# A mask, a scan and the matmul order of the attention loop, moved on four engines

## The reference, cut to what matters

```python
for t in range(S):                       # S = 768; B*H = 32 heads of D = 48
    cur = einsum('bhd,bhe->bhde', u * k[t], v[t])
    y[t] = einsum('bhd,bhde->bhe', r[t], state + cur)
    state = w[t][..., None] * state + einsum('bhd,bhe->bhde', k[t], v[t])
x = y.transpose(0, 2, 1, 3).reshape(B * S, H * D)     # 3072 x 384
x = moe(x)          # skip gate, argmax over 8 experts, relu(x @ w1) @ w2
return moe2(x)      # softmax over tokens and over slots, 8 experts
```

## Time and profile before

| What | us |
|---|---|
| three runs | 380.25, 381.19, 381.48 |
| median | 381.19 |
| profiled execution: its span, first to last instruction | 387.5 |
| attention, to the first transpose of a token tile (L637) | 138.3 |
| one pair of attention once the loop has settled | 8.10 |

### The profile page before, as it was taken

One profiled execution on the slowest core, in us unless ns is written; L12 is line 12 of the kernel. 1 busy time (PEld: TensorE's weight loads), 2 busy tenths in 40 slices (PEclk: granted clock), 3 DMA queues, 4 the chain that ended last, 5 costly groups with the idle time before them and its releaser, 6 DMA issues.

```text
span 387.5 us, 14814 instructions
## 1 busy us (share of the span) xinstructions
PE 354.1 (91%) x5880; PEld 269.6 (70%) x5880; DVE 281.8 (73%) x564; ACT 221.0 (57%) x681; POOL 115.0 (30%) x179
## 2 busy tenths in 40 slices
PE   6699999999999999889999999999999999679990
PEld 6487777877777788656777777777777777345360
DVE  7999999999999634786676767777677776430371
ACT  3777888778887755134656556565555664200060
POOL 3543322343223340254222233332221224540000
PEclk9989999999999999989999999999999999689996
DMA  8987656766568995013193799495858779759438
GB/s 310 415 305 265 241 198 216 257 258 248 197 205 286 424 402 205 3 23 111 29 393 128 300 323 393 178 361 193 325 211 321 263 259 396 281 170 327 167 152 336
DMA packets 31300, 97.58 MB, mean 252 GB/s; under 512 B 4062, under 2 KB 14410, under 8 KB 29722
## 3 DMA queue, kind: packets, MB, share of 16 engines
q1 hardware_dynamic: 29466, 93.81, 65.2%
q0 software_dynamic: 1792, 3.17, 2.7%
HBM read 85.53 MB, written 11.45 MB: 250 GB/s over the span
## 4 chain that ended last, share of the span: by engine, by line
PE 56%; DVE 5%; another core or an unknown queue 3%; issue 1%; POOL 1%; ACT 1%; DVEq 0%; ACTq 0%
PE a_bank L772 19%; PE y_bank L781 18%; PE y_bank L928 3%; PE a_bank L944 3%; PE a_bank L637 2%; DVE x_all L1550 2%; PE sums_bank L705 1%; PE a_bank L832 1%; PE y_bank L598 1%; PE y_bank L593 1%; PE ktok_bank L645 1%; PE sums_bank L645 1%; PE y_bank L605 1%; PE y_bank L740 0%
## 5 line engine op out<-in xcount | busy, mean ns | idle before, releaser
L781 PE MATMUL y_bank<-w_sb,work 128*32 128x192 f32 x1664 | 78.5, 326 | 0.5 <-ACT work L1131 0.5
L772 PE MATMUL a_bank<-w_sb,work 128*32 128x256 f32 x1248 | 77.9, 382 | 0.1
L781 PEld LDWEIGHTS y_bank<-w_sb,work 128*32 128x32 f32 x1664 | 64.9, 110 | 8.8 <-DVE work L1396 1.1
L1586 POOL TENSOR_SCALAR_AFFINE_SELECT a_sb<-a_sb 128x512 f32<-128x512 f32 x48 | 44.2, 932 | 86.7 <-ACT a_sb L1016 86.7
L772 PEld LDWEIGHTS a_bank<-w_sb,work 128*32 128x32 f32 x1248 | 42.4, 109 | 25.6 <-issue 13.0
L1026 ACT ACTIVATE bonus_v<-v_sb,bonus 128x48 f32<-128x48 f32 x192 | 45.0, 321 | 14.0 <-DVE x_all L1260 13.9
L1104 ACT ACTIVATE work<-work 32x96 f32<-32x96 f32 x108 | 30.4, 281 | 39.3 <-PE a_bank L772 37.0
L1440 DVE TENSOR_TENSOR ys<-work 32x192 f32<-32x192 f32 x104 | 37.0, 355 | 9.9 <-ACT work L1131 9.2
L1396 DVE STREAM_TRANSPOSE work<-hid 128x256 f32<-128x256 f32 x53 | 23.6, 446 | 26.2 <-PE y_bank L781 22.9
L572 PE MATMUL a_bank<-r_in,k_in 64*128 64x128 f32 x384 | 31.0, 295 | 0.1
L572 PEld LDWEIGHTS a_bank<-r_in,k_in 64*128 64x128 f32 x384 | 24.7, 193 | 6.3 <-issue 5.7
(11 more groups left out here) (314 smaller groups left out, 582.6 us busy)
## 6 DMA issues: line engine op xcount, KB each, us to landing
w_sb<-in_moe_w SPq DMA_DIRECT2D x20, 1536.0 KB, 11.7
wrk_sb<-in_wrk SPq DMA_DIRECT2D x16, 768.0 KB, 7.0
e_sb<-in_moe_w SPq DMA_DIRECT2D x8, 1536.0 KB, 11.0
wrk_sb<-in_wrk SPq DMA_DIRECT2D x15, 780.0 KB
v_sb<-in_vt SPq DMA_DIRECT2D x16, 288.0 KB, 2.9
tokens<-x_all SPq DMA_DIRECT2D x4, 1152.0 KB, 21.7
out<-x_all SPq DMA_DIRECT2D x12, 384.0 KB, 3.9
x_all<-in_moe_w SPq DMA_DIRECT2D x2, 1536.0 KB
```

Of the source, the lines that this page charges most:

```text
L772: last = nc.tensor.matmul(out[SUB * g:SUB * (g + 1), 0:FB], x[:, kk, :], w1_sb[j][:, kk, FB * g:FB * (g + 1)], start=(kk == 0), stop=(kk = ...
L781: last = nc.tensor.matmul(bank[4][SUB * g:SUB * (g + 1), 0:YW], h_t[:, SUB * k:SUB * (k + 1)], w2_sb[j][:, k, d:d + YW], start=(b == 0), s ...
L1586: nc.gpsimd.affine_select(out=x, in_=x, compare_op=ALU.is_gt, fill=0.0, base=0, pattern=[[0, 2], [0, 2], [1, C]], channel_multiplier=-1).t ...
```

## The change

It has five parts. (a) GpSimd masks the scores of a pair in one operation of 1536 elements per partition in place of three of 512, and waits for all three copies of the pair and, but for the last pair, for `mid_w_ready` of the next pair. (b) VectorE's second scan is taken out of `products` as `mid_down` and stands behind `x_out` and `chain`, and ahead of `k_input`. (c) TensorE's order within a pair is new: y_transposes right behind k_transposes, the bonus rows behind the second scores, chunk_sums ahead of bonus_turned. (d) The bonus rows go to the upper half of `ktok_bank` instead of a place in `a_bank`; they wait for the copy of that bank, and their own copy no longer waits for `a_full`. (e) ScalarE copies all three scores in a row, then the bonus rows, and `spread_mid_w` moves from the head of a pair to behind them.

```diff
--- before.py
+++ after.py
@@ -342,9 +342,7 @@
         WHOLE = HALF
         y_cols = y_bank[:, :, :].rearrange("p b t -> p (b t)")[:, 0:S]
 
-        def bonus_cols(g):
-
-            return a_bank[:, 2 * (g % 2), 2 * C:4 * C]
+        bonus_cols = ktok_bank[:, 2 * C:4 * C]
 
 
         def half_rows(t, h0, h1, backwards):
@@ -546,9 +544,8 @@
                 nc.tensor.transpose(sums_bank[:, NC * D:NC * D + C], k_in[:, c * C:(c + 1) * C], ident[:, :]).then_inc(ktok_full, 1)
 
             def bonus_rows(n):
-                out = bonus_cols(3 * n + 1)
-                if n:
-                    pe.wait_ge(a_copied, 3 * n)
+                pe.wait_ge(ktok_copied, 2 * n + 1)
+                out = bonus_cols
                 for c in range(NC):
                     i = c % 4
                     last = nc.tensor.matmul(out[32 * i:32 * i + 32, c // 4 * C:(c // 4 + 1) * C], u_sb[:, n % QP, :], rk[:, c * C:(c + 1) * C],
@@ -592,7 +589,7 @@
                         rows = slice(64 * a, 64 * a + 64)
                         nc.tensor.matmul(y_cols[64 * a:64 * a + D, c * C:(c + 1) * C], state[n % 2][rows, :, c - 1], r_in[n % 3][rows, c * C:(c + 1) * C],
                                          start=(c in (1, 4)), stop=False, tile_position=(64 * a, 64 * a), skip_group_check=True)
-                pe.wait_ge(a_masked, 3 * n + 3)
+                pe.wait_ge(a_masked, n + 1)
                 for c in range(NC):
                     for a in range(2):
                         last = nc.tensor.matmul(y_cols[64 * a:64 * a + D, c * C:(c + 1) * C], v_sb[n % 4][:, c, a, :], a_sb[n % 2][:, a, c, :],
@@ -611,17 +608,16 @@
             pe.wait_ge(dummy_clear, 1)
             for n in range(PAIRS):
                 k_transposes(n)
+                if n >= 2:
+                    y_transposes(n - 2)
                 pe.wait_ge(r_ready, n + 1)
                 a_products(n, 0)
+                a_products(n, 1)
                 pe.wait_ge(rk_ready, n + 1)
                 bonus_rows(n)
-                a_products(n, 1)
                 a_products(n, 2)
-                if n >= 2:
-                    y_transposes(n - 2)
-                pe.wait_ge(ktok_copied, 2 * n + 1)
+                chunk_sums(n)
                 bonus_turned(n)
-                chunk_sums(n)
                 if n:
                     y_products(n - 1)
 
@@ -1000,8 +996,7 @@
 
             def copy_bonus_rows(n):
                 act.wait_ge(bonus_full, 2 * n + 1)
-                act.wait_ge(a_full, 3 * n + 2)
-                nc.scalar.activation(bonus_ch, bonus_cols(3 * n + 1), ACT.Copy).then_inc(bonus_copied, 1)
+                nc.scalar.activation(bonus_ch, bonus_cols, ACT.Copy).then_inc(bonus_copied, 1)
 
             def copy_bonus(n):
                 act.wait_ge(bonus_full, 2 * n + 2)
@@ -1034,21 +1029,21 @@
                                      ACT.Copy).then_inc(mid_rows_ready, 1)
 
             act.wait_ge(tables_begun, 2)
-            for t, n in ((sums_bank[:, :], 4 * P), (a_bank[:, 0, 2 * C:], 2 * P), (a_bank[:, 2, 2 * C:], 2 * P), (y_cols, S)):
+            for t, n in ((sums_bank[:, :], 4 * P), (y_cols, S)):
                 last = nc.scalar.activation(t, ones_at[:, 0:n], ACT.Copy, scale=0.0)
             last.then_inc(dummy_clear, 1)
             act.wait_ge(tables_begun, 3)
             act.sem_inc(y_parts_ready, 1)
             act.sem_inc(h_ready, 1)
             for n in range(PAIRS):
-                spread_mid_w(n)
                 if n >= 2:
                     copy_y(n - 2)
                 copy_ktok(n)
                 copy_a(n, 0)
-                copy_bonus_rows(n)
                 copy_a(n, 1)
                 copy_a(n, 2)
+                copy_bonus_rows(n)
+                spread_mid_w(n)
                 copy_bonus(n)
                 weigh_v(n)
 
@@ -1215,11 +1210,13 @@
                 V.tensor_tensor_scan(decay[:, 0:SCAN], wrk_sb[i][:, 0:SCAN], ones_at[:, :], 0.0, ALU.mult, ALU.add).then_inc(mid_up_ready, 1)
 
             def products(n):
-                i = n % 3
                 rows = decay[:, :].rearrange("p (g m) -> p g m", m=ROW)
                 dve.wait_ge(mid_up_ready, n + 1)
                 V.reciprocal(inv_at[:, :].rearrange("p (g m) -> p g m", m=ROW)[:, :, 0], rows[:, 0:2 * NC, WHOLE]).then_inc(inv_ready, 1)
                 V.tensor_tensor(mid_w[n % 2][:, :], rows[:, NC:2 * NC - 1, WHOLE], rows[:, 1:NC, WHOLE], ALU.mult).then_inc(mid_w_ready, 1)
+
+            def mid_down(n):
+                i = n % 3
                 dve.wait_ge(inv_ready, n + 1)
                 if n == 0:
                     dve.wait_ge(ld_small, 16)
@@ -1270,6 +1267,7 @@
             dve.wait_ge(tables_begun, 3)
             mid_up(0)
             products(0)
+            mid_down(0)
             k_input(0)
             r_inputs(0)
             for n in range(1, PAIRS):
@@ -1277,8 +1275,9 @@
                 products(n)
                 if n >= 3:
                     x_out(n - 3)
+                chain(n - 1)
+                mid_down(n)
                 k_input(n)
-                chain(n - 1)
                 r_inputs(n)
 
             def gate_copies(q):
@@ -1580,11 +1579,12 @@
             nc.gpsimd.iota(name[:, :], pattern=[[1, NT]], base=-NOWHERE, channel_multiplier=LINE, **kw).then_inc(tables_ready, 1)
 
             for n in range(PAIRS):
-                for s in range(3):
-                    pool.wait_ge(a_copied, 3 * n + s + 1)
-                    x = a_sb[n % 2][:, :, 2 * s:2 * s + 2, :]
-                    nc.gpsimd.affine_select(out=x, in_=x, compare_op=ALU.is_gt, fill=0.0, base=0,
-                                            pattern=[[0, 2], [0, 2], [1, C]], channel_multiplier=-1).then_inc(a_masked, 1)
+                pool.wait_ge(a_copied, 3 * n + 3)
+                if n < PAIRS - 1:
+                    pool.wait_ge(mid_w_ready, n + 2)
+                x = a_sb[n % 2][:, :, :, :]
+                nc.gpsimd.affine_select(out=x, in_=x, compare_op=ALU.is_gt, fill=0.0, base=0,
+                                        pattern=[[0, 2], [0, NC], [1, C]], channel_multiplier=-1).then_inc(a_masked, 1)
 
             pool.sem_inc(weight_there, 1)
             pool.sem_inc(stage_turned, 1)
```

## The result

The changed kernel takes 392.2 us (median of four runs, 390.6 to 393.2) where the kernel before, beside it on the same chip, takes 380.9. The ratio is 1.031, with a 95% interval of 1.027 to 1.034: slower, by 11.3 us. The forecast was 395.2, in a range of 389 to 400.5.

What follows compares the result with a forecast made beforehand. VectorE was taken to set the pace now, and a closed ring plus the mask's hold after the change, 9.03 us a pair. 1.5 + 0.85 + 0.9 + 1.0 + 11.2 - 1.4 = +14.0 on 381.2 gives 395.2 us, range 389 to 400.5.

Steps and rivals of the forecast that it cites:

- The ring: Closed chain from k_in through TensorE, ScalarE and the state scan to the next k_in: 8.83 us a pair against 8.10.
- the hold: GpSimd's mask keeps VectorE's second scan from K + 6.97 to K + 7.17, making 9.03 us a pair.
- The mask: GpSimd's single mask of 1536 elements: begins 5.75 us behind k_in, takes 1.57, ends at K + 7.32.
- the first rival: The mask doesn't hold the second scan and a ring of 8.83 remains: +11.0, 392.2 us; chance 0.20.
- The hiding place: Mask beside x_out and state scan: it ends at K + 7.32, while the second scan could start at K + 6.97.
- The sum: Attention loop's first steps, twelve settled pairs and the end behind the sixteenth k_in, together +14.0 us.
- The twelve settled pairs: Attention loop behind the fourth k_in: 12 x 0.93 = 11.2 us longer.
- The first steps: From first to fourth k_in: +1.5, then +0.85 and about 0.9 for TensorE's low clock, then +1.0 us.
- The lag of TensorE behind the last k_in: Sixteenth k_in to first token transpose: K + 9.2 at the latest where it was K + 10.53, -1.4 us.
- the sentence that ScalarE comes in time for the next y_transposes: ScalarE's weigh_v and copy_y were said to come ahead of TensorE's next y_transposes; no size given.
- The third rival: TensorE's clock may fall more often with a gap in each pair: adds 5.4, 400.6 us; chance 0.08.
- the 6.3 us between span and median: Profiled span of 387.5 lies 6.3 above the runs' median of 381.2, taken to hold for both kernels.

Runs made afterwards that it cites:

- three_masks: The changed kernel with three masks of 512, each behind its copy, and all the new orders kept: 395.5 us against 387.5, ratio 1.021.
- spread_early: The changed kernel with one edit, ScalarE spreads mid_w right behind the copy of k_tok instead of behind the bonus rows: 391.4 us, ratio 1.029.
- state_scan_ahead: The kernel before with one mask waiting for the next pair's second scan, and the state scan between x_out and k_in: ratio 1.000.
- one_mask_alone: The kernel before with one mask of 1536 and both its waits, all orders as before: 393.5 us against 389.3, ratio 1.011.
- vector_order_back: The changed kernel with VectorE's second scan ahead of x_out and k_in ahead of the state scan again: 387.4 us, ratio 1.018.

## Why the prediction was right, and where its sizes were off

**The ring** was the mechanism. Its length without the hold was forecast at 8.83 and was 8.57, the sum of the terms below less 0.14; three_masks ran at 8.56. Term by term, in us, the measured ones from the timeline of the changed kernel:

| Term | forecast | measured |
|---|---|---|
| k_in to k_transposes | 1.10 | 1.01 |
| k_transposes | 0.70 | 0.60 |
| y_transposes | 0.71 | 0.75 |
| two scores | 1.20 | 1.09 |
| bonus rows | 0.55 | 0.56 |
| third scores to their copy | 0.83 | 0.76 |
| copy | 0.50 | 0.50 |
| bonus copy | 0.28 | 0.26 |
| spreading and hand-over | 0.43 | 0.51 |
| state scan | 0.67 | 0.67 |
| second scan to k_in | 1.86 | 2.00 with the hold |

The first six terms came out 0.32 too long in all. Where two groups of TensorE follow each other and the shape of the product changes, the change is in the step, and in the new order other groups meet: k_transposes took 0.70 ahead of scores and takes 0.60 ahead of other transposes. That this explains all of the 0.32 is not shown. The hand-over to VectorE, 0.04, was a guess. From the end of the spreading (66.70) to the state scan it is 0.10. VectorE waits 0.70 a pair there, for the 1.01 forecast.

**The mask** was forecast at 1.57 and is 1.55, begins 5.44 behind k_in for 5.75, and holds the second scan by 0.14 for 0.20. The rule cited from the Trainium skill (SBUF — State Buffer, "SBUF: two separate sides"), that the lock is kept for the whole instruction, would have held it to the mask's very end, 67.75. The trace differs a little: by its length of 1.91 the scan got under way at 67.61. That a scan can be held at all, which was the first rival's doubt, spread_early settled: 2.45.

**The hiding place.** The window of x_out and state scan was said to close before the mask is through. It does, and state_scan_ahead shows that this holds even without the ring: from the end of the second scan to k_in it is 1.23 there, for 0.13 to start the mask and 1.55 of work less the 0.14 at its end.

**The sum** was 14.0 and the end of attention moved by 9.65. The twelve settled pairs gave 7.4 for 11.2 (12 times 0.62 for 0.93); this is the term that was mis-sized, by 0.26 a pair in the ring and 0.06 in the hold. The first steps were forecast at +1.5, +1.75 and +1.0 and came at +1.4, +2.15 and +0.7; the second holds TensorE's low clock (granted 0.50 from 18 to 21.2 us, behind a gap of 3.60), which cost more than 0.9, since two scores (2.08 for 1.16) were hit beside the bonus rows (1.07 for 0.63):

```profile
18.15 2.08 PE L569 MATMUL a_bank<-r_in,k_in 64*128 64x128 f32 x16
...
20.15 1.07 PE L551 MATMUL ktok_bank<-work,u_sb 128*32 128x128 f32 x12
...
25.89 0.96 DVE L1237 TENSOR_TENSOR k_in<-wrk_sb,decay 128x768 f32<-128x768 f32 x1
```

The lag of TensorE behind the last k_in was 8.78 for 10.53, so -1.75 where -1.4 stood, and the first k_in came 0.2 earlier, as no transfer was waited for. The median moved by 11.3, nearer to the forecast than the profiles' 9.65; part of that nearness is luck. It is luck too that the measured 392.2 is the very number of the first rival. That rival had no hold and a ring of 8.83, and the runs show a hold and a ring of 8.57.

**Not foreseen** was the second round of 8.40 through copy_y. It lies 0.3 below the ring, so it could not show in the changed kernel; but it was there to be counted in the sentence that ScalarE comes in time for the next y_transposes, which gave no number. The third rival did not come: TensorE's granted clock was 1.00 from 40 to 160 us, with a gap of 0.88 in each pair.

**Taken wrongly** was the 6.3 us between span and median as something common to both kernels. It came of the waits behind the experts described above, which the other profiled execution doesn't have. The sum was added to the median and not to the span, so the forecast did not suffer.

## What to carry to other kernels

Before an operation of an engine is moved ahead of another, follow the loop once round through the other engines. Here TensorE's work on k_in lagged behind for free as long as the state scan, which needs it, stood behind the next k_in. It was on the path as soon as the state scan stood ahead. An operation that has to fit a narrow window should not wait for the semaphore that opens it, where its data are there earlier anyway: here that wait cost 0.3 us of k_in in each pair, and 0.15 of the pace. A busy share of 99% names the engine that binds now, not the floor that comes next; here a round of 7.85 through TensorE and ScalarE, another of 8.40 through the same two and a ring of 8.56 through three stood close by.

## What the runs showed of the hardware

In these traces a VectorE operation with two SBUF inputs, product or scan, and a mask on GpSimd keep each other waiting, and each is let in a little before the other ends. The profile shows the waiting as a longer operation and not as idle time before it: 1.27, 1.59 and 1.26 for a k_in of 0.96, 2.45 for a scan of 1.77, 2.01 for a mask of 1.55. The mask lets the scan in 0.14 (67.75 less 67.61) and 0.13 (spread_early) before its end. The second scan of one_mask_alone ends at 64.09 and the mask behind it at 65.43, so that its 1.55 of work began at 63.88, 0.21 before. In vector_order_back it is 0.15: k_in ends at 66.49, and the mask of 1.80 at 67.89. These margins are worked out from lengths, with nothing else to check them by.

Operations of VectorE that read one input from PSUM kept their length beside a mask: x_out 0.72 to 0.76, the state scan 0.74 to 0.76. A mask of 1536 elements took 1.55, where one of 512 took 0.64, one of 128 0.29 and one of 8 0.19.
